# A clustered-attention head pipeline on one core: masks turned between two heads, the similarity step one unit earlier, and 16-bit cluster marks

## What is computed

```
q_assign = argmax(q_n @ c_n.T)      # nearest of 16 centroids, per head
k_assign = argmax(k_n @ c_n.T)
mask   = q_assign[:, None] == k_assign[None, :]
scores = where(mask, q @ k.T / 8, -1e9)
attn   = exp(scores - max(scores)) / (sum + 1e-9)
out    = attn @ v
```

## Time and profile before

| | before |
|---|---|
| median of 3 runs | 846.76 us (845.66 to 849.64) |
| the profiled execution | 848.11 us, of which the span of instructions is 846.3 us |
| PE, PEld, DVE busy in the span | 95%, 88%, 69% |
| ACT, POOL busy | 58%, 33% |
| mean granted TensorE clock | 0.993 of full speed |

### The profile page before, as it was taken

How to read it: one execution, slowest core, us unless ns; L and a number is a source line. 1 busy time by engine, 2 the same in 40 slices (tenths; PEclk the granted TensorE clock), 3 DMA queues, 4 the chain that set the end, 5 groups by cost and what they waited for, 6 DMA issues and landing times.

```text
span 846.3 us, 13234 instructions
## 1 busy us (share of the span) xinstructions
PE 803.2 (95%) x4339; PEld 748.7 (88%) x4339; DVE 580.9 (69%) x970; ACT 492.2 (58%) x836; POOL 275.2 (33%) x292
## 2 busy tenths in 40 slices
PE   5889999999999999999999999988999999999996
PEld 4778888888889999999999999977998998998995
DVE  6678878887876343343343344468888888888885
ACT  2357666677668611121111123368999999999995
POOL 4436677667668589300000016660000000000000
PEclk9999999999999999999999999999999999999999
DMA  6433644645533234100000004430001001001001
GB/s 178 129 98 107 171 107 121 147 101 146 130 82 79 70 106 125 64 0 0 0 0 0 0 4 129 128 89 1 1 2 37 0 0 37 0 0 37 1 1 37
DMA packets 30316, 52.15 MB, mean 62 GB/s; under 512 B 9184, under 2 KB 11328, under 8 KB 30272
## 3 DMA queue, kind: packets, MB, share of 16 engines
q1 hardware_dynamic: 30272, 51.59, 22.6%
HBM read 29.40 MB, written 3.19 MB: 39 GB/s over the span
## 4 chain that ended last, share of the span: by engine, by line
PE 78%; DVE 12%; ACT 5%; issue 3%; POOL 1%; DMA 1%; POOLq 0%; ACTq 0%; DVEq 0%; SPq 0%
PE ps L192 28%; PE ps L982 15%; PE ps L990 13%; PE ps L603 5%; DVE row_max L864 4%; PE ps L636 3%; PE ps L664 3%; PE ps L647 3%; PE ps L580 3%; PE ps L665 3%; PE ps L672 3%; DVE eq L850 2%; ACT scratch L1034 1%; ACT scratch L1040 1%; PE ps L591 1%
## 5 line engine op out<-in xcount | busy, mean ns | idle before, releaser
L198 ACT ACTIVATE g_hi<-g_f 128x384 fp32r<-128x384 f32 x128 | 67.4, 527 | 219.0 <-PE ps L982 201.3
L210 DVE TENSOR_SCALAR corr<-ps,alpha_c 128x384 f32<-128x384 f32 x64 | 39.5, 617 | 136.0 <-PE ps L192 135.9
L744 ACT ACTIVATE probs_hi<-ps 128x768 fp32r<-128x768 f32 x96 | 78.1, 813 | 88.4 <-PE ps L647 87.7
L192 PE MATMUL ps<-x_lo,w_hi_b 128*128 (+1 forms) x352 | 118.8, 337 | 0.0
L192 PE MATMUL ps<-x_hi,w_hi_b 128*128 (+1 forms) x352 | 118.7, 337 | 0.0
L192 PE MATMUL ps<-x_hi,w_lo_b 128*128 (+1 forms) x352 | 118.7, 337 | 0.0
L864 DVE TENSOR_REDUCE row_max<-ps 128x1 fp32r<-128x768 f32 x96 | 90.8, 948 | 35.8 <-PE ps L603 35.4
L343 POOL TENSOR_TENSOR probs_lo<-probs,probs_hi 128x768 fp32r<-128x768 f32 x32 | 58.9, 1840 | 93.6 <-ACT probs L747 93.6
L202 DVE TENSOR_TENSOR g_lo<-g_f,g_hi 128x384 fp32r<-128x384 f32 x128 | 76.5, 598 | 0.6 <-ACT g_hi L198 0.6
L343 DVE TENSOR_TENSOR probs_lo<-ps,probs_hi 128x768 fp32r<-128x768 f32 x64 | 60.8, 950 | 18.0 <-ACT ps L747 18.0
L603 PE MATMUL ps<-op_a 128*128 128x384 f32 x192 | 56.5, 379 | 16.2 <-DVE row_max L864 13.3
(11 more groups left out here) (129 smaller groups left out, 2100.1 us busy)
## 6 DMA issues: line engine op xcount, KB each, us to landing
stage<-in_moe_w_in SPq DMA_DIRECT2D x27, 256.0 KB, 2.6
stage<-in_moe_w_out SPq DMA_DIRECT2D x27, 256.0 KB, 2.9
raw<-in_qk SPq DMA_DIRECT2D x16, 384.0 KB, 3.8
op_a<-head_hi SPq DMA_DIRECT2D x32, 192.0 KB, 3.6
v_raw<-in_v SPq DMA_DIRECT2D x16, 192.0 KB, 2.4
op_b<-head_hi SPq DMA_DIRECT2D x16, 192.0 KB, 3.7
op_b<-head_lo SPq DMA_DIRECT2D x16, 192.0 KB, 3.9
scratch<-spread SPq DMA_DIRECT2D x16, 192.0 KB, 5.2
```

Source lines behind the costliest of these rows:

```text
L192: last = pe.matmul(h_ps[j % H_RING][:, 0:BLK], a[:, 0, w], x[:, kt, cols], start=(kt == 0 and i == 0), stop=(kt == KT - 1 and i == 2))
L198: act.activation(g_hi[:, j % 2], g_f[:, j % 2], ACT.Copy).then_inc(g_hi_made, 1)
L744: act.activation(probs_hi[:, g % P_RING], scores(g), ACT.Exp, scale=SCALE).then_inc(exp_hi_made, 1)
```

## The change

- `onehot`'s inputs `rank`, `eq` and `first_rank` become bf16.
- The turned masks of head 3 and later go into bank 4, columns 0 to 383, rows 0 to 63 (those of heads 1 and 2 stay in bank 7, that of head 0 moves to bank 4 too), instead of the spare columns of banks 2 to 4. The copies into `op_a` read one run of 768 instead of three of 256.
- `turn_onehot(n+3)` stands at the end of unit 5 of head n, behind `weigh_lo`, instead of unit 0 of head n+1 ahead of `score`. It waits for `take_pv(n, 0)`.
- `put_mask_k(n+3)` follows ACT's exponentials of unit 5 of head n. `put_mask_q` stays in unit 0 of the next head, and no longer waits for that unit's exponential. The score matmuls of unit 2 no longer wait for the masks; the first `weigh_hi` still does.
- `sim(n+3)` and `nearest(n+3)` move from unit 2 to unit 1; `guard` of tile 5 in unit 2 now waits until `nearest` has emptied the similarity's columns.
- `ranked` and the reduce of `first_nearest` stay in unit 3. The mark becomes `mark_nearest`, in unit 4 behind DVE's `make_lo`.

```
-            rank = sba("rank", [P, C])
+            rank = sba("rank", [P, C], BF16)
-            eq = sba("eq", [P, T, 2, C])
-            first_rank = sba("first_rank", [P, T, 2])
+            eq = sba("eq", [P, T, 2, C], BF16)
+            first_rank = sba("first_rank", [P, T, 2], BF16)
...
+            def masks(m, r, rows_=32):
+                return ps[r * 32:r * 32 + rows_, 7 if m in (1, 2) else 4, 0:HS].bitcast(BF16)
...
# PE, sim(m)
-                        pe.wait_ge(guard_taken, (T, T + 2)[m - 2] if m < 4 else T * (m - 1) - 1)
+                        pe.wait_ge(guard_taken, (T, T + 2, 2 * T + 3)[m - 2] if m < 5 else T * (m - 1) - 2)
# PE, turn_onehot(m)
                     if m >= 3:
-                        pe.wait_ge(pv_taken, 2 * (m - 2) - 1)
+                        pe.wait_ge(pv_taken, 2 * (m - 3) + 1)
# PE, guard(m, t)
+                def sims_before(m, t):
+                    if m < 2:
+                        return 1 if m == 0 else 3 if t < TH else 4
+                    return min(m + (3 if t >= (4 if m == 2 else 5) else 2), N)
...
-                    pe.wait_ge(sim_taken, 1 if m == 0 else 3 if m == 1 and t < TH else min(max(m, 2) + 2, N))
+                    pe.wait_ge(sim_taken, sims_before(m, t))
# PE, scores_free(g)
-                    if before >= 0 and u == 0 and n >= 1 and n + 2 < N:
-                        pe.wait_ge(mask_q_put, n + 3)
-                        pe.wait_ge(mask_k_put, n + 3)
# PE, prepare(n, s) and the unit loop
-                    elif s == 2 and n + 3 < N:
+                    elif s == 1 and n + 3 < N:
                         sim(n + 3)
...
-                        if s == 0 and n >= 1 and n + 2 < N:
-                            turn_onehot(n + 2)
...
+                        if s == U - 1 and n + 3 < N:
+                            turn_onehot(n + 3)
# ACT
-                    if n >= 1 and s == 0 and n + 2 < N:
-                        put_mask_k(n + 2)
+                    if s == U - 1 and n + 3 < N:
+                        put_mask_k(n + 3)
# DVE
+                def mark_nearest(m):
                     dve.wait_ge(onehot_step, 3 * m + 3)
                     at_least(dve, onehot_turned, m)
...
-                    if m >= 3:
-                        dve.wait_ge(exp_made, (m - 2) * U + 1)
...
-                    if n == 0 and s in (1, 3) or n >= 1 and s == 2 and n + 3 < N:
+                    if n == 0 and s in (1, 3) or n >= 1 and s == 1 and n + 3 < N:
                         nearest(n + 3 if n else 2 + s // 3)
...
+                    if n == 0 and s in (1, 4) or n >= 1 and s == 4 and n + 3 < N:
+                        mark_nearest(n + 3 if n else 2 + s // 4)
```

More of the change, by code:

```diff
@@ L290, in by_bank @@
                 return ap.rearrange("p (a t) x -> p a (t x)", a=2)
[L294 to L303, removed]
+            def masks(m, r, rows_=32):
+                return ps[r * 32:r * 32 + rows_, 7 if m in (1, 2) else 4, 0:HS].bitcast(BF16)
             def mask_rows(m, side):
-                return op_a[64:96, m % 3, side].rearrange("p (a n) -> p a n", a=TH)
+                return op_a[64:96, m % 3, side]
             def max_at(m, rows_=T):
@@ L588, in turn_onehot @@
                     if m >= 3:
-                        pe.wait_ge(pv_taken, 2 * (m - 2) - 1)
+                        pe.wait_ge(pv_taken, 2 * (m - 3) + 1)
                     for t in range(T):
-                        last = pe.transpose(turned(m, t), onehot[:, t].rearrange("p x c -> p (x c)"), ident_b[:])
+                        last = pe.transpose(masks(m, 0, 64)[:, t * P:(t + 1) * P], onehot[:, t].rearrange("p x c -> p (x c)"), ident_b[:])
                     last.then_inc(onehot_turned, 1)
+                def sims_before(m, t):
+                    if m < 2:
+                        return 1 if m == 0 else 3 if t < TH else 4
+                    return min(m + (3 if t >= (4 if m == 2 else 5) else 2), N)
                 def guard(m, t):
@@ L891, in _ @@
                 first_nearest(0)
+                mark_nearest(0)
                 for e in range(2):
@@ L901, in _ @@
                 first_nearest(1)
+                mark_nearest(1)
                 set_op_b(1)
```

## The result

| | before | after |
|---|---|---|
| median | 846.98 us (845.66 to 849.64, 4 runs) | 838.91 us (837.20 to 839.74, 4 runs) |
| ratio, 95% interval | | 0.9898 (0.9870 to 0.9927) |
| profiled execution, its span | 848.11, 846.3 us | 838.85, 837.1 us |

What follows compares the result with a forecast made beforehand. PE was taken to bound the kernel, standing 2.3 us per head. Gains of 1.7 (six heads), 2.0 (five), 0.6 (head 12 to 13) and 1.2 (16 bits) made 5.5 us: median 841.3, range 832 to 849.

Steps and rivals of the forecast that it cites:

- step 5: ranked in 16 bits: only the 0.21 us behind POOL's end can shrink; 0.1 gained in each of 12 heads.
- step 3: Units 0 to 2: put_mask_q ends earlier and the wait before the first weigh_hi goes; 0.43 us gained, bounds 0.34 and 0.43.
- Step 1: Units 3 to 5: the mark leaves the path, ranked stays blocked; guard of unit 5 at 149.22 in place of 149.61.
- Step 2: End of unit 5: PE stands 0.49 us for the mark before turn_onehot; 0.15 gained in even heads, 0.26 in odd.
- step 4: sim and nearest a unit earlier: 0.29 us lost to a wait before guard of unit 2, replacing 0.35 before turn_max.
- rival A: Unit 3: ranked comes ahead of POOL, DVE's chain runs 1.25 us earlier; 6.0 more gained, 835.3 us; chance 0.20.
- rival D: Slower: the mark meets the start of a POOL instruction, with PE's queue behind it; 851.7 us; chance 0.10.
- B: Rival: 16-bit operands are not held by POOL at all; 13.2 us more gained, 828.1 us; chance 0.08.
- C: Rival: nothing gained; 0.25 of "issue" returns at the new place, guard of unit 2 waits longer; 846.1 us; chance 0.20.

Runs made afterwards that it cites:

- The last kernel: The changed kernel with mark ahead of make_lo, turn_onehot and put_mask_k in unit 0, guard of unit 2 behind weigh_lo, head 1's sim and nearest in unit 2: 831.18 us.

## Why the prediction was right in direction and short in size

Each part added in turn gives the spacing per head, in the profiled executions:

| kernel | per head | step | forecast |
|---|---|---|---|
| before | 16.52 | | |
| 16 bits | 16.42 | -0.10 | -0.1 (step 5) |
| and bank 4, waits dropped | 16.13 | -0.29 | -0.43 (step 3) |
| and turn at the end of unit 5, mark in unit 4 | 15.90 | -0.23 | -0.15 or -0.26 (steps 1, 2) |
| and similarity in unit 1: the change | 15.68 | -0.22 | +0.29 (step 4) |

- **What bounds** was right: PE's loads are busy the same, and all of the gain is idle time of PE.
- **Step 1 failed, on its assumption.** "I assume that `ranked` is still blocked" holds for the first three parts (it is held in each of them, for 1.34 to 1.52) and not for the change: from head 2 to 12 it starts between 0.01 ahead of POOL and 0.04 behind, and takes 0.23. It is rival A, in even heads too, where I had it in odd ones only in the sum.
- **Step 4 failed in one sentence, and that is the cause.** I wrote of the 0.35 before `turn_max` that it goes "but this brings nothing", because DVE is pinned to POOL. DVE is behind POOL because it is late by that wait, which ACT and POOL don't have; without it DVE is first. Per head the step was forecast as 0.29 lost and gave 0.22, which is 0.51 and more than all of the difference between 0.84 and 0.44. The loss that step 4 did count is there: 0.35 before `guard` of unit 2, for 0.29. What it left out is in PE's waits of the two kernels, with the similarity in unit 2 and in unit 1, per head: for `row_max` 0.49 and nothing, `turn_max` 0.35 and nothing, "issue" before `guard` 0.17 and 0.35, for the mark 0.59 and 1.02. The sum is 0.23 less, and the spacing is 0.22 less.
- **Step 2** was right that the turn would stand for the mark, and how it would: its 0.49 is 0.48 in an even head with the similarity in unit 2 (mark at 114.31, turn at 114.71), and 0.95 in head 5. In the change it is 1.13: DVE comes 1.3 us earlier, and meets the beginning of `w_lo_a` in place of its end. This is rival D's mechanism, as part of A, and D's sign, a mark of over 1 us in most heads, is there without D's loss. POOL's start is pinned to ACT, and DVE's no longer to POOL's end, which is what D's "against" had relied on. A's own figure for the even heads had the mark done 4.5 behind POOL's start; it was 4.07 (146.17 less 142.10). In the odd heads A had it done at 3.4, behind the first L512, and 1.2 gained. That came about in heads 5 and 9 only (3.5 and 3.6); in 3, 7 and 11 it was 4.1, because one L504 takes 1.01 and not half of 2.21, so that the second had begun 0.12 before the mark was asked for. That is why A's 6.0 more didn't come. That the wait for `take_pv` "costs nothing" holds for the change, and ceases to hold once the mark is early: PE stands 0.86 in head 5 and 1.25 in head 9.
- **Step 3** was right in kind and 0.14 too large. The stand before the first `weigh_hi` is 0.40 on average over the 11 heads, 0.43 in the earlier trace rows being the usual one, and with the masks' bank and waits alone about 0.10 of it stays; the load still starts 0.22 behind `put_mask_q` (0.26 before). So 0.30 is gained there, just under the lower bound of 0.34. In the change PE comes to this load later, behind `sim`, and doesn't stand at all.
- **Head 1** I took as nothing "within one wait of 1 us". It lost about that. At the same mean granted clock up to it (0.94), `turn_max` of head 1 is at 61.98 in the change and at 61.21 with the similarity in unit 2. Over all kernels at 0.94 it is at 61.51 to 62.00 with the similarity in unit 1 and at 61.21 and 61.46 with it in unit 2; at 0.97 at 61.09 and 59.85. So the loss is between 0.1 and 1.2. PE stands 1.74 before a `guard` there, where it stood at most 1.02 with the similarity in unit 2.
- **The other rivals.** B is out, as the mark in 16 bits is held for 1.07 and 1.50. C's first half, the return of the 0.25, can't be seen in the change, where the stand for the mark covers it; it is there at the new place in the kernels with the mark ahead of `make_lo` (0.25 in most heads) or in unit 3 (0.26). The interval excludes no gain.
- **The end of the attention.** Head 12 takes 14.23 in place of 14.69, where 0.7 was forecast, and head 13 takes 13.06 in place of 12.62. The sum had no term for the last.

From `turn_max` of head 1 on it comes to 9.24 + 0.46 - 0.44 = 9.26 less, minus 0.52 in head 1 is 8.74, and 0.5 more behind head 14 is the span's 9.2. The medians' 8.1 is 1.2 less than the 9.26 of the profiled executions, and 1.13 of that is what the one of before lay above its median.

What stays open is how much of the early mark's gain the total keeps. Its stretch is 5.6 us shorter than the change's; its median is 4.4 less, and by the two ratios to the kernel before, each run beside it, 5.2 less. In the profiled executions it comes to `turn_max` of head 1 1.5 later, at a lower clock, and takes 0.7 longer behind head 12's; why the latter, isn't shown.

## What to carry to other kernels

An instruction held "by" another engine can be a race that one side loses by a few tenths (0.47 us here): look for what makes the loser late, in the rows before both, ahead of assuming that it will always lose. An instruction that is freed early runs into the next holder, so find its place in the gap between two of them (here ahead of `make_lo`, not behind it). And when a wait moves together with the queue that stands behind it, price the two apart: turning the masks between the heads lost 0.47 us per head in the change's order (0.15 with the mark ahead), and the change was still faster.

## What the runs showed of the hardware

**The hold has a margin, and it depends on what POOL did before.** `ranked` (two SBUF inputs) meets POOL's subtraction L335, before which POOL stands (0.74 us in head 6 of the change). Over the heads of all kernels it was not held when its record started up to 0.05 us behind that of POOL, and up to 0.11 with the memset in front, and was held for the whole of it at 0.15 (1.81 us, head 9 above), 0.24 (1.71) and from 0.43 on. When the two started level, POOL's instruction grew from 1.84 to between 1.93 and 2.09; with DVE 0.27 or more ahead it stayed at 1.84. Where POOL's instruction follows another one at once, there was no such margin: the mark was held for the whole of the second L504 when it started 0.12 behind it (1.08, heads 3, 7 and 11 of the change), and even at 0.02 (1.21, head 3 of the kernel with the turn alone in unit 0). The Trainium skill (SBUF — State Buffer, Who interferes with whom) says that the lock is exclusive and that issue order decides who blocks; both cases here agree, with the addition that the order of the recorded starts isn't that order within some 0.1 us. The records are not that sharp themselves: the memset's overlaps that of `ranked` by 0.07.

**The clock at the start.** TensorE's granted clock between 30 and 50 us was 0.66 to 1.00 of full speed in the profiled executions, for nearly the same work: 0.83 before and after, 0.66 in the kernel with the mark ahead, 1.00 in the last one. It is a mix of the two levels, 1.2 and 2.4 GHz: a pair of loads of `score` takes 0.65 us in one stretch and 0.36 in the other. Some kernels have a stretch at the lower level after 50 us instead or as well. The last kernel, and the one with the turn alone in unit 0 up to its `turn_max` of head 1:

```profile
30.00:50.00 20.00, 16.74 (x88) 13.78 (x87) 14.81 (x22) 8.29 (x12) 5.76 (x6) 1.00 0.38 96
```
```profile
50.00:64.28 14.28, 12.07 (x54) 11.18 (x55) 9.53 (x12) 5.75 (x8) 6.24 (x7) 0.76 0.54 143
```

The columns are length, busy times, granted clock, DMA share, GB/s. `turn_max` of head 1 comes the later, the lower the mean granted clock from the start up to it. With head 1's similarity in unit 2 it was at 59.63 and 59.78 (clock 1.00), 59.85 (0.97), 61.21 and 61.46 (0.94) and 62.19 (0.92). With it in unit 1 it was at 61.09 (0.97), 61.51, 61.98 and 62.00 (0.94), and 63.48, 63.78 and 64.28 (0.89); the 64.28 is the kernel with the turn alone in unit 0. So some 2 us of a total are decided before most of the edits matter, and the spacing of the heads is the sharper measure.
